# Routing logits of four token tiles: products summed on VectorE instead of transposes and products on TensorE

## The chip, the cores and the metric

One core of a Trainium2 chip runs the whole program. The metric is the device time of one execution in microseconds (us). Times inside an execution are counted from its first instruction. PE is TensorE, DVE is VectorE, ACT is ScalarE, POOL is GpSimd, and SP is the engine that issues most DMAs.

## The reference, cut to what matters

An attention with a hash mask gives x (1536 tokens of 512 numbers). A first mixture of 8 experts, weighted with Sinkhorn-normalised gates, gives a new x. The second mixture sends each token of this new x to one expert:

```python
xn = x / (np.linalg.norm(x, axis=-1, keepdims=True) + 1e-06)
en = expert_emb / (np.linalg.norm(expert_emb, axis=-1, keepdims=True) + 1e-06)
logits = xn @ en.T / tau                     # [1536, 8]
expert_idx = np.argmax(logits, axis=1)
probs = softmax(logits)
out[mask] = gate_w[mask, None] * (np.maximum(x[mask] @ w1[e], 0.0) @ w2[e])
```

The change concerns the logits of the second mixture, for tokens 0 to 511 in the kernel's tile order: 8 dot products of length 512 for each token.

## The kernel before, in words

Tokens lie in 12 tiles of 128 (TT); the first mixture works on three chunks of four tiles (CH = 3, CT = 4). The attention takes the first 250 us. Then each expert e of the first mixture does for each chunk c: the **up** product, 8 blocks f of 12 matmuls into the four PSUM banks 0 to 3 in turn; ACT takes the relu of each block (`h_hi`, L1302) and DVE the rounding rest (`h_lo`, L1737), which frees the bank. Then the **down** product, 32 pairs j of 3 matmuls into banks 4 to 7, after which DVE adds the scaled result to the four token rows (`tok`, L1800). Every fp32 product is three matmuls of rounded parts (`matmul_x3`, L476 to L480). PE holds the order of work: its instructions are written out by hand in one queue, and small products of the second mixture's routing are put between the matmuls of the last expert (e = 7).

In chunk 1 of the last expert these are the routing steps of tiles 0 to 3, whose rows are final by then. `tokens_beside` (L935) puts them before the pairs j = 7t, 7t + 3, 7t + 6 and 7t + 9 of the down product:

- `turn_token` (L909): four 128x128 transposes of the token rows into bank 0. ACT copies them to `x_t` and squares the rows for the norm (`token`, L1254).
- `token_logits` (L917): four fp32 products of `x_t` and the turned embeddings `emb_t` into bank 1.
- `token_rank` (L923): waits until DVE has chosen the expert (`s_chosen`), then two small bf16 products.
- `table_part` (L928): waits for a table cell from DVE (`s_cell`).

DVE's side is `choose` (L1646: six small instructions from the logits to the chosen expert, the running counts and a copy of the logits), then `find_cell` (L1660), then two blocks of `w2_lo` (L1723), four times (L1759 to L1767), all behind the eight `h_lo` of that chunk. On DVE, `link` (L1390) makes the engine wait for the completion of each such instruction before the next. ACT's side is, after its eight relus, `token(t, 0)` and two blocks of `w2_hi2` (L1291) for each of the four tiles (L1310 to L1313); `w2_hi2` writes the second mixture's first weights over the xt arrays.

```python
    pe.wait_ge(s_chosen, t + 1)                                  # token_rank, L924
    pe.matmul(psum[:, bank, 0:E], prior[:], chosen[:], start=True, stop=False)
```

SP loads the weights of each expert as they come free; near the end of the first mixture it issues the load of `w2_raw` (L433), and then the stores of finished token rows to `x_rows` (L435 to L453).

The last tiles (4 to 11) are routed in chunk 2 of the last expert and behind it, with the same functions. After that come the 19 or so token tiles of the second mixture (`tiles2`).

Of the kernel before, what the change touches and what calls it, by code (L numbers as in the profile page):

```python
# [13 lines left out]
P = 128  # L14
# [13 lines left out]
def program(nc, q, k, v, proj, w_gate, w1, w2, emb, tau, m2w1, m2w2, out):  # L28
# [7 lines left out]
    TT = N // P  # L36
# [36 lines left out]
    x_t = place("x_t", [P, KD, P], F32, gate_t_at)  # L73
    emb_sq = gate_t[0:E, :]
# [47 lines left out]
    assert N == 1536 and FF == 1024 and DM == 512  # L122
    left = [[dead + 4 * (kd * N + 1024)] for kd in range(4)]
# [106 lines left out]
    x_rows = nc.dram_tensor("x_rows", [N, DM], F32).ap()  # L230
    weights = nc.dram_tensor("weights", [N, 1], F32).ap()
# [3 lines left out]
    s_turned, s_copied, s_logits = sem("token_turned"), sem("token_copied"), sem("token_logits")  # L235
    s_chosen, s_rank, s_cell = sem("token_chosen"), sem("token_rank"), sem("token_cell")
# [121 lines left out]
    def _(sp):  # L358
# [65 lines left out]
        with sp.Fori(0, E - 1) as e:  # L424

            sp.wait_ge(m1.w1_lo, e + 1)
            sp.dma_start(w1_raw[:], m1.wa[e + 1]).then_inc(m1.w1_in, 16)
            sp.wait_ge(m1.w2_lo, KF * (e + 1))
            sp.dma_start(w2_raw[:], m1.wb[e + 1]).then_inc(m1.w2_in, 16)
        sp.wait_ge(m1.w1_lo, E)  # L430
        sp.dma_start(w1_raw[:], m2.wa[0]).then_inc(m2.w1_in, 16)
        sp.wait_ge(m1.w2_lo, KF * E)
        sp.dma_start(w2_raw[:], m2.wb[0]).then_inc(m2.w2_in, 16)  # L433

# [13 lines left out]
        sp.wait_ge(s_turned, 2 * CT)  # L448
# [265 lines left out]
    def _(pe):  # L714
# [194 lines left out]
        def turn_token(t, bank):  # L909
            pe.wait_ge(m1.y, (E - 1) * TT + t + 2)  # L910
            if t > 0:
                pe.wait_ge(s_squares, t)
            for kd in range(KD):
                tr = pe.transpose(psum[:, bank, kd * P:kd * P + P], tok[:, t, kd * P:kd * P + P], ident[:])
            tr.then_inc(s_turned, 1)

        def token_logits(t, bank):  # L917
            pe.wait_ge(s_copied, t + 1)
            for kd in range(KD):
                mm = pe.matmul(psum[:, bank, 0:E], x_t[:, kd, :], emb_t[:, kd, :], start=(kd == 0), stop=(kd == KD - 1))  # L920
            mm.then_inc(s_logits, 1)
# [13 lines left out]
        def tokens_beside(j, n):  # L935

            for t in range(CT):
                if j == 7 * t:
                    if t == 0:
                        pe.wait_ge(m1.h_lo, KF * n + 4 + 5)  # L940
                    turn_token(t, 0)
                if j == 7 * t + 3:
                    if t == 0:
                        pe.wait_ge(m1.h_lo, KF * n + 5 + 5)
                    token_logits(t, 1)
                if j == 7 * t + 6:
                    if t == 0:
                        pe.wait_ge(m1.h_lo, KF * n + 6 + 5)
                    token_rank(t, 2)
                if j == 7 * t + 9:  # L950
                    if t == 0:
                        pe.wait_ge(m1.h_lo, KF * n + 7 + 5)
                    table_part(t, 3)
# [122 lines left out]
        for kd in range(KD):  # L1076
            if kd % 2 == 0:
                pe.wait_ge(s_copied, TT + kd // 2)
            mm = pe.matmul(psum[:, 1, 0:E], x_t[:, kd, :], emb_t[:, kd, :], start=(kd == 0), stop=(kd == KD - 1))
# [70 lines left out]
    def _(act):  # L1150
# [103 lines left out]
        def token(t, bank):  # L1254

            if t > 0:
                act.wait_ge(s_logits, t)
            act.wait_ge(s_turned, t + 1)
            act.copy(x_t[:].rearrange("p k i -> p (k i)"), psum[:, bank, :]).then_inc(s_copied, 1)
            act.wait_ge(s_copied, t + 1)  # L1260
            act.activation(psum[:, bank, :], tok[:, t, :], ACT.Square,
                           accum_out=per_tok[:, 0, t:t + 1]).then_inc(s_squares, 1)

        def last_token():
            t = TT - 1
            act.wait_ge(s_logits, t)
            act.wait_ge(s_turn_half, 1)
            act.copy(x_t[:, 0:2, :].rearrange("p k i -> p (k i)"), psum[:, 0, 0:256]).then_inc(s_copied, 1)
            act.wait_ge(s_turned, TT)
            act.copy(x_t[:, 2:4, :].rearrange("p k i -> p (k i)"), psum[:, 7, 0:256]).then_inc(s_copied, 1)  # L1270
            act.wait_ge(s_copied, TT + 1)
            act.activation(psum[:, 0, :], tok[:, t, :], ACT.Square,
                           accum_out=per_tok[:, 0, t:t + 1]).then_inc(s_squares, 1)
# [22 lines left out]
        def expert(e, first=False, last=False):  # L1296
            for c in range(CH):
# [12 lines left out]
                if last and c == 1:  # L1310
                    for t in range(CT):
                        token(t, 0)
                        w2_hi2(0, 0, w2_raw, (2 * t, 2 * t + 1))  # L1313
# [73 lines left out]
    def _(dve):  # L1387
# [258 lines left out]
        def choose(t, bank):  # L1646

            dve.wait_ge(s_logits, t + 1)
            scores_, best = psum[:, bank, 0:E], per_tok[:, 4, t:t + 1]
# [6 lines left out]
            link(dve.tensor_copy(logit[:, t, :], scores_))  # L1656
            if t == TT - 1:
                dve.sem_inc(s_total_in, 1)

# [72 lines left out]
        def expert(e, first=False, last=False):  # L1732
            for c in range(CH):
                n = CH * e + c
                for f in range(KF):
# [5 lines left out]
                    if first and c == 1:  # L1741
# [8 lines left out]
                        if 2 <= f < 2 + CT:  # L1750
                            first_y(f - 2)
                    if last and c == 2:
# [173 lines left out]
```

## Time and profile before

| | |
|---|---|
| median of 3 runs | 1570.8 us (1570.76 to 1570.91) |
| the profiled execution's own time | 1570.5 us |
| its span, first to last instruction | 1568.6 us |
| PE busy | 1545.6 us (99%) |
| DVE busy | 686.0 us (44%) |
| ACT busy | 516.0 us (33%) |
| POOL busy | 332.3 us (21%) |
| share of the chain that ended last on PE | 96% |
| mean granted clock of PE | 0.995 |

Busy time counts an instruction from its start to its end. Neighbouring matmuls overlap in it (each lasts 0.39 us and starts 0.23 us after the last), so the distance from start to start is what a matmul costs; the same is true of two DVE instructions with no wait between them. A granted clock of 1.00 is 2.4 GHz on TensorE, 0.50 is 1.2 GHz.

### The profile page before, as it was taken

Reading aid. Unit: us, or ns where it says so; the run is one execution under the profiler, and the core shown is the slowest. Engines: PE = TensorE matmul, PEld = TensorE weight load, DVE = VectorE, ACT = ScalarE, POOL = GpSimd, SP = SyncE. Lnnn points to the kernel's source line nnn. Section 1 sums busy time; section 2 is a strip of 40 time slices with the busy share of each in tenths; the row PEclk is TensorE's granted clock in tenths of the full one; section 3 lists DMA queues with packets and bytes.
Section 4 is the critical chain, followed back from the end, with each engine's and each line's share of the span. In section 5 each row is a group of like instructions: output and inputs, shape, how many; then the busy total and the mean of one; then the engine's idle time right before and its main releaser. Section 6 shows DMA issues by size and latency. Waiting matters only on the chain.

```text
span 1568.6 us, 21673 instructions
## 1 busy us (share of the span) xinstructions
PE 1545.6 (99%) x7493; PEld 1292.6 (82%) x7494; DVE 686.0 (44%) x1242; ACT 516.0 (33%) x946; POOL 332.3 (21%) x563
## 2 busy tenths in 40 slices
PE   8999999999999999999999999999999999999997
PEld 7999997888888888888888888888888888788886
DVE  7999985423222311311322221121132255887665
ACT  6888885012111101101211111011121133676554
POOL 4565656000300300120030030012004000233222
PEclk9999999999999999999999999999999999899999
DMA  6545561101100200110110011011011122774310
GB/s 164 136 113 144 124 179 55 54 1 54 55 1 1 80 27 0 53 53 0 53 54 0 0 68 39 0 53 53 0 38 69 41 81 75 251 260 163 118 40 25
DMA packets 44775, 108.88 MB, mean 69 GB/s; under 512 B 5782, under 2 KB 7830, under 8 KB 44736
## 3 DMA queue, kind: packets, MB, share of 16 engines
q1 hardware_dynamic: 41088, 99.83, 20.4%
q0 software_dynamic: 3424, 8.14, 1.6%
q8 instruction: 24, 0.39, 0.1%
q10 hardware_dynamic: 224, 0.39, 0.1%
q14 instruction: 15, 0.12, 0.0%
HBM read 81.57 MB, written 8.13 MB: 57 GB/s over the span
## 4 chain that ended last, share of the span: by engine, by line
PE 96%; DVE 2%; ACT 1%; issue 1%; POOL 0%; DVEq 0%; POOLq 0%; ACTq 0%
PE psum L478 27%; PE psum L479 26%; PE psum L480 26%; PE psum L786 4%; PE psum L773 2%; PE psum L800 2%; PE psum L799 2%; PE psum L774 2%; PE psum L1113 1%; PE psum L754 1%; PE psum L813 1%; PE psum L920 1%; PE psum L1104 0%; ACT prob L1169 0%; DVE pt_lo L1431 0%
## 5 line engine op out<-in xcount | busy, mean ns | idle before, releaser
L1302 ACT ACTIVATE h_hi<-psum 128x512 fp32r<-128x512 f32 x192 | 114.9, 598 | 878.5 <-PE psum L480 878.5
L478 PE MATMUL psum<-w_lo,h_hi 128*128 128x512 f32 x768 | 304.4, 396 | 0.0
L479 PE MATMUL psum<-w_hi,h_hi 128*128 128x512 f32 x768 | 302.5, 394 | 0.0
L478 PE MATMUL psum<-xt_lo,w_hi 128*128 128x512 f32 x768 | 300.3, 391 | 0.0
L479 PE MATMUL psum<-xt_hi,w_hi 128*128 128x512 f32 x768 | 299.0, 389 | 0.0
L480 PE MATMUL psum<-xt_hi,w_lo 128*128 128x512 f32 x768 | 298.9, 389 | 0.0
L480 PE MATMUL psum<-w_hi,h_lo 128*128 128x512 f32 x768 | 298.5, 389 | 0.0
L1737 DVE SCALAR_TENSOR_TENSOR h_lo<-psum,h_hi 128x512 fp32r<-128x512 f32 x192 | 133.0, 693 | 351.3 <-ACT h_hi L1302 351.3
L1800 DVE SCALAR_TENSOR_TENSOR tok<-psum,route,tok 128x512 f32<-128x512 f32 x83 | 56.8, 745 | 358.6 <-PE psum L480 358.6
L509 POOL CAST w_hi<-w_raw 128x512 fp32r<-128x512 f32 x68 | 41.6, 611 | 802.0 <-PE psum L480 801.6
L480 PEld LDWEIGHTS psum<-w_hi,h_lo 128*128 128x128 f32 x768 | 144.2, 188 | 32.5
L478 PEld LDWEIGHTS psum<-w_lo,h_hi 128*128 128x128 f32 x768 | 144.2, 188 | 32.1
L480 PEld LDWEIGHTS psum<-xt_hi,w_lo 128*128 128x128 f32 x768 | 144.2, 188 | 30.1
L478 PEld LDWEIGHTS psum<-xt_lo,w_hi 128*128 128x128 f32 x768 | 144.2, 188 | 29.8
L479 PEld LDWEIGHTS psum<-xt_hi,w_hi 128*128 128x128 f32 x768 | 144.2, 188 | 29.4
L479 PEld LDWEIGHTS psum<-w_hi,h_hi 128*128 128x128 f32 x768 | 144.6, 188 | 27.4
L1431 DVE TENSOR_TENSOR pt_lo<-psum,pt_hi 128x384 fp32r<-128x384 f32 x192 | 97.5, 549 | 18.4 <-ACT pt_hi L1162 17.7
L1169 ACT ACTIVATE prob<-psum,row_bias,row_scale 128x768 f32<-128x768 f32 x96 | 95.9, 999 | 20.4 <-POOL row_bias L558 18.6
L1441 DVE TENSOR_REDUCE row_min<-psum 128x1 f32<-128x768 f32 x96 | 90.8, 947 | 1.1 <-PE psum L774 0.7
L1162 ACT CAST pt_hi<-psum 128x384 fp32r<-128x384 f32 x192 | 83.0, 486 | 14.1 <-PE psum L786 12.9
L631 POOL TENSOR_TENSOR w_lo<-w_raw,w_hi 128x512 fp32r<-128x512 f32 x64 | 82.6, 1291 | 12.5 <-issue 7.2
L786 PE MATMUL psum<-ident,prob 128*128 128x128 f32 x576 | 80.7, 275 | 2.2 <-DVE pt_lo L1431 1.7
(272 smaller groups left out, 1996.0 us busy)
## 6 DMA issues: line engine op xcount, KB each, us to landing
w_raw<-in_moe_w_dram SPq DMA_DIRECT2D x25, 2048.0 KB, 8.2
w_raw_odd<-in_moe_w_dram SPq DMA_DIRECT2D x4, 2048.0 KB, 10.3
k_hh<-k_hi SPq DMA_DIRECT2D x32, 192.0 KB, 3.0
w_raw_even<-in_moe_w_dram SPq DMA_DIRECT2D x3, 2048.0 KB, 9.2
x_rows<-tok SPq DMA_DIRECT2D x14, 256.0 KB, 2.4
k_raw<-in_k_dram SPq DMA_DIRECT2D x8, 384.0 KB, 3.1
v_raw<-in_v_dram SPq DMA_DIRECT2D x16, 192.0 KB, 3.4
q_b<-q_hi SPq DMA_DIRECT2D x16, 192.0 KB, 4.0
```

What stands on the lines that cost most here:

```text
L478: pe.matmul(acc, a[0], b[1], start=start, stop=False)
L479: pe.matmul(acc, a[0], b[0], start=False, stop=False)
L480: return pe.matmul(acc, a[1], b[0], start=False, stop=stop)
L631: pool.tensor_tensor(w2_s[1][:, f, :], w2_raw[:, f, :], w2_s[0][:, f, :].bitcast(F32), ALU.subtract).then_inc(m1.w2_lo, 1)
L786: tr = pe.transpose(psum[:, 4 + c, j * P:j * P + P], prob[par][:, 3 * c + j, :], ident[:])
L1162: act.copy(pt_hi[half][:, 3 * c:3 * c + 3, a:a + P], psum[:, 4 + c, 0:HALF].rearrange("p (j i) -> p j i", j=3)).then_inc((s_hi_a, s_hi_b)[ ...
L1169: act.activation(prob[t % 2][:].rearrange("p (c j) i -> p c (j i)", c=2), psum[:, score_bank(g, t):score_bank(g, t) + 2, 0:HALF], ACT.Exp, ...
L1302: act.activation(h_s[0][:, f, :], psum[:, f % 4, :], ACT.Relu).then_inc(m1.h_hi, 1)
L1431: dve.tensor_tensor(pt_lo[half][:, 3 * c:3 * c + 3, a:a + P], psum[:, 4 + c, 0:HALF].rearrange("p (j i) -> p j i", j=3), pt_hi[half][:, 3 ...
L1441: dve.tensor_reduce(row_min[:, c], psum[:, score_bank(g, t):score_bank(g, t) + 2, 0:HALF], AX.XY, ALU.min).then_inc(s_min, 1)
L1737: dve.scalar_tensor_tensor(h_s[1][:, f, :], psum[:, f % 4, :], 0.0, h_s[0][:, f, :].bitcast(F32), ALU.max, ALU.subtract).then_inc(m1.h_lo, 1)
L1800: dve.scalar_tensor_tensor(tok[:, tile, 0:DM], psum[:, 4 + i, :], route[:, e, tile:tile + 1], tok[:, tile, 0:DM], ALU.mult, ALU.add).then_ ...
```

## The change

The eight normalised embedding rows (16 KB, made early in the first mixture) are stored to a scratch tensor in device memory, and read back into every one of the 128 partitions (`emb_all`, 8 x 512 numbers per partition, 2 MB). `emb_all` lies over the columns of the xt arrays that chunk 0 used, so SP issues the read once the last expert's up product of chunk 0 is done. Then DVE computes, for tiles 0 to 3, each of the 8 logits with one instruction: the product of the 128 token rows with one repeated embedding row, with the sum over the 512 products put out beside it (`accum_out`). Four such linked instructions follow each `h_lo` of chunk 1 of the last expert: 32 in all. The transposes, the copies and the TensorE products of tiles 0 to 3 go; ACT's squares stay and wait for nothing of PE. ACT's `w2_hi2`, which writes over `emb_all`, waits until all four tiles' dot products are done (`s_dots`). `choose` reads the sums instead of PSUM and has no logits to copy. The counts of `s_turned`, `s_copied` and `s_logits` shift by 4.

```diff
     x_t = place("x_t", [P, KD, P], F32, gate_t_at)
+    dot_terms = x_t[:].rearrange("p k i -> p (k i)")
     emb_sq = gate_t[0:E, :]
...
     assert N == 1536 and FF == 1024 and DM == 512
+    assert 2 * KD == E
+    emb_all = place("emb_all", [P, E, N], F32, [dead])
     left = [[dead + 4 * (kd * N + 1024)] for kd in range(4)]
...
     x_rows = nc.dram_tensor("x_rows", [N, DM], F32).ap()
+    emb_rows = nc.dram_tensor("emb_rows", [E, DM], F32).ap()
     weights = nc.dram_tensor("weights", [N, 1], F32).ap()
...
     s_turned, s_copied, s_logits = sem("token_turned"), sem("token_copied"), sem("token_logits")
+    s_emb_stored, s_emb_all, s_dots = sem("emb_rows_stored"), sem("emb_broadcast_loaded"), sem("token_dots")
     s_chosen, s_rank, s_cell = sem("token_chosen"), sem("token_rank"), sem("token_cell")
...
             sp.dma_start(w2_raw[:], m1.wb[e + 1]).then_inc(m1.w2_in, 16)
+        sp.wait_ge(s_emb_ready, 1)
+        sp.dma_start(emb_rows, emb_sq).then_inc(s_emb_stored, 16)
         sp.wait_ge(m1.w1_lo, E)
...
         sp.dma_start(w2_raw[:], m2.wb[0]).then_inc(m2.w2_in, 16)
+
+        sp.wait_ge(s_emb_stored, 16)
+        sp.wait_ge(m1.up, KF * (CH * (E - 1) + 1) + 1)
+        sp.dma_start(emb_all[:, :, 0:512], emb_rows.partition_broadcast(P)).then_inc(s_emb_all, 16)
...
         sp.wait_ge(s_x_stored, 16 * 2 * CT)
-        sp.wait_ge(s_turned, 2 * CT)
+        sp.wait_ge(s_turned, CT)
         sp.wait_ge(s_squares, 2 * CT)
...
             pe.wait_ge(m1.y, (E - 1) * TT + t + 2)
-            if t > 0:
-                pe.wait_ge(s_squares, t)
+            pe.wait_ge(s_squares, t)
             for kd in range(KD):
...
         def token_logits(t, bank):
-            pe.wait_ge(s_copied, t + 1)
+            pe.wait_ge(s_copied, t - CT + 1)
             for kd in range(KD):
...
             for t in range(CT):
-                if j == 7 * t:
-                    if t == 0:
-                        pe.wait_ge(m1.h_lo, KF * n + 4 + 5)
-                    turn_token(t, 0)
-                if j == 7 * t + 3:
-                    if t == 0:
-                        pe.wait_ge(m1.h_lo, KF * n + 5 + 5)
-                    token_logits(t, 1)
                 if j == 7 * t + 6:
...
-            if t > 0:
-                act.wait_ge(s_logits, t)
-            act.wait_ge(s_turned, t + 1)
-            act.copy(x_t[:].rearrange("p k i -> p (k i)"), psum[:, bank, :]).then_inc(s_copied, 1)
-            act.wait_ge(s_copied, t + 1)
+            if t < CT:
+                act.wait_ge(m1.y, (E - 1) * TT + t + 2)
+                if t > 0:
+                    act.wait_ge(s_squares, t)
+            else:
+                if t > CT:
+                    act.wait_ge(s_logits, t - CT)
+                act.wait_ge(s_turned, t - CT + 1)
+                act.copy(x_t[:].rearrange("p k i -> p (k i)"), psum[:, bank, :]).then_inc(s_copied, 1)
+                act.wait_ge(s_copied, t - CT + 1)
             act.activation(psum[:, bank, :], tok[:, t, :], ACT.Square,
...
             t = TT - 1
-            act.wait_ge(s_logits, t)
+            act.wait_ge(s_logits, t - CT)
             act.wait_ge(s_turn_half, 1)
             act.copy(x_t[:, 0:2, :].rearrange("p k i -> p (k i)"), psum[:, 0, 0:256]).then_inc(s_copied, 1)
-            act.wait_ge(s_turned, TT)
+            act.wait_ge(s_turned, TT - CT)
             act.copy(x_t[:, 2:4, :].rearrange("p k i -> p (k i)"), psum[:, 7, 0:256]).then_inc(s_copied, 1)
-            act.wait_ge(s_copied, TT + 1)
+            act.wait_ge(s_copied, TT - CT + 1)
             act.activation(psum[:, 0, :], tok[:, t, :], ACT.Square,
...
                 if last and c == 1:
+                    act.wait_ge(m1.h_lo, KF * n + 4 + 5)
                     for t in range(CT):
                         token(t, 0)
+                        if t == 0:
+                            act.wait_ge(s_dots, CT)
                         w2_hi2(0, 0, w2_raw, (2 * t, 2 * t + 1))
...
-            dve.wait_ge(s_logits, t + 1)
-            scores_, best = psum[:, bank, 0:E], per_tok[:, 4, t:t + 1]
+            if t < CT:
+                dve.wait_ge(s_dots, t + 1)
+            else:
+                dve.wait_ge(s_logits, t - CT + 1)
+            scores_ = logit[:, t, :] if t < CT else psum[:, bank, 0:E]
+            best = per_tok[:, 4, t:t + 1]
             link(dve.tensor_reduce(best, scores_, AX.X, ALU.max))
...
             link(dve.tensor_tensor(counts[:, (t + 1) % 2, :], counts[:, t % 2, :], chosen[:], ALU.add))
-            link(dve.tensor_copy(logit[:, t, :], scores_))
+            if t >= CT:
+                link(dve.tensor_copy(logit[:, t, :], scores_))
             if t == TT - 1:
                 dve.sem_inc(s_total_in, 1)
+
+        def token_dots(t, experts):
+
+            dve.wait_ge(s_emb_all, 16)
+            dve.wait_ge(m1.y, (E - 1) * TT + t + 2)
+            for e in experts:
+                link(dve.scalar_tensor_tensor(dot_terms, tok[:, t, :], 1.0, emb_all[:, e, 0:512], ALU.mult, ALU.mult,
+                                              accum_out=logit[:, t, e:e + 1]))
+            if E - 1 in experts:
+                dve.sem_inc(s_dots, 1)
...
                             first_y(f - 2)
+                    if last and c == 1:
+                        token_dots(f // 2, range(f % 2 * E // 2, (f % 2 + 1) * E // 2))
                     if last and c == 2:
```

## Rows read from the trace of the kernel before

**Rows 1.** Busy time and clock by stretch: chunk 1 up and chunk 1 down, last expert.
```profile
core 0: us, PE busy (x) PEld busy (x) DVE busy (x) ACT busy (x) POOL busy (x), PEclk, DMA share, GB/s
1228.00:1249.80 21.80, 21.80 (x97) 17.99 (x97) 8.97 (x19) 4.19 (x7) 0.00 (x0) 1.00 0.19 72
1249.80:1278.20 28.40, 28.40 (x157) 23.25 (x155) 15.75 (x58) 9.86 (x21) 0.00 (x0) 1.00 0.01 1
```

**Rows 2.** The chain that ended last, chunk 1 down: start us, us, what.
```profile
1249.98 0.44 PE psum L914 x4
...
1252.49 0.79 PE psum L920 x8
1253.28 0.34 PE psum L478
```

**Rows 3.** PE in order of time, last expert: start us, us, engine, line.
```profile
1206.08 0.39 PE L478 MATMUL psum<-w_lo,h_hi 128*128 128x512 f32 x1
...
1228.05 0.39 PE L478 MATMUL psum<-xt_lo,w_hi 128*128 128x512 f32 x1
...
1255.06 0.40 PE L480 MATMUL psum<-w_hi,h_lo 128*128 128x512 f32 x1
1255.30 0.18 PE L925 MATMUL psum<-chosen,prior 128*128 128x8 bf16 x1
```

**Rows 4.** DVE in order of time, chunk 1 of the last expert.
```profile
1232.68 0.69 DVE L1737 SCALAR_TENSOR_TENSOR h_lo<-psum,h_hi 128x512 fp32r<-128x512 f32 x1
...
1253.31 0.17 DVE L1650 TENSOR_REDUCE per_tok<-psum 128x1 f32<-128x8 f32 x1 [1.97 <-PE psum L920]
...
1257.24 1.30 DVE L1726 TENSOR_TENSOR xt_lo<-w_raw,xt_hi 128x512 fp32r<-128x512 f32 x2
```

**Rows 5.** DVE in order of time, first expert: two unlinked instructions, then two linked ones.
```profile
320.80 0.69 DVE L1737 SCALAR_TENSOR_TENSOR h_lo<-psum,h_hi 128x512 fp32r<-128x512 f32 x1 [1.29 <-ACT h_hi L1302]
321.40 0.74 DVE L1729 TENSOR_SCALAR tok<-psum,route 128x512 f32<-128x512 f32 x1
...
332.28 0.67 DVE L1623 TENSOR_TENSOR gate_t<-emb_raw 8x512 f32<-8x512 f32 x1
332.99 0.67 DVE L1624 TENSOR_REDUCE one_col<-gate_t 8x1 f32<-8x512 f32 x1
```

**Rows 6.** DVE's groups, shapes apart: xcount, busy us, mean ns, idle before.
```profile
L1421 DVE TENSOR_TENSOR k_lo<-k_raw,k_hi 128x768 fp32r<-128x768 f32 x1 | 1.0, 957 | 0.1
L1423 DVE SCALAR_TENSOR_TENSOR q_lo<-q_raw,q_hi 128x768 fp32r<-128x768 f32 x1 | 1.0, 957 | 0.1
...
L1664 DVE TENSOR_REDUCE spot<-pick 128x1 f32<-128x8 f32 x12 | 1.9, 162 | 0.4
```

**Rows 7.** ACT in order of time: a sum's readout, two blocks of w2_hi2.
```profile
1251.67 0.19 ACT L1261 ACTIVATION_READ_ACCUMULATOR psum<-tok 128x1 f32 x1
1251.76 1.12 ACT L1294 CAST xt_hi<-w_raw 128x512 fp32r<-128x512 f32 x2
```

**Rows 8.** DVE in order of time: the last tile's choice begins.
```profile
1338.29 0.17 DVE L1650 TENSOR_REDUCE per_tok<-psum 128x1 f32<-128x8 f32 x1 [0.34 <-DVE tab L1821]
```

**Rows 9.** PE in order of time: the last tile's rank product, which waited for that choice.
```profile
1339.30 0.18 PE L925 MATMUL psum<-chosen,prior 128*128 128x8 bf16 x1 [0.92 <-DVEq L1654]
```

**Rows 10.** Busy time and clock by stretch, columns as in rows 1, after the last expert.
```profile
1338.00:1342.00 4.00, 2.46 (x18) 1.91 (x16) 2.64 (x15) 1.70 (x3) 0.84 (x4) 0.94 0.97 295
1342.00:1346.00 4.00, 2.56 (x12) 1.77 (x10) 2.59 (x11) 0.58 (x1) 0.22 (x2) 0.50 0.53 206
1346.00:1350.00 4.00, 4.00 (x10) 3.13 (x11) 2.29 (x8) 2.65 (x6) 1.44 (x3) 0.50 0.29 72
```

**Rows 11.** PE in order of time where its clock is at half and comes back.
```profile
1346.53 0.63 PE L479 MATMUL psum<-w_hi,x_hi 128*128 128x512 f32 x1
...
1351.96 0.39 PE L480 MATMUL psum<-w_hi,x_lo 128*128 128x512 f32 x1
```

**Rows 12.** DMA issues, 1195 to 1215 us: xcount, KB each, median us to landing.
```profile
w_raw<-in_moe_w_dram SPq DMA_DIRECT2D x1, 2048.0 KB, 8.4
```

More of the change, by code:

```diff
@@ L1077, in _ @@
             if kd % 2 == 0:
-                pe.wait_ge(s_copied, TT + kd // 2)
+                pe.wait_ge(s_copied, TT - CT + kd // 2)
             mm = pe.matmul(psum[:, 1, 0:E], x_t[:, kd, :], emb_t[:, kd, :], start=(kd == 0), stop=(kd == KD - 1))
```

## The prediction

> **What bounds the kernel now.** I read the page first: PE is busy for 99% of the span and the chain that ended last is 96% PE, so whatever leaves PE's queue shortens the run and whatever stops PE lengthens it. Then the busy times by stretch, for the place of the change [rows 1]: in chunk 1 of the last expert the up product takes 21.8 us and the down product 28.4 us, PE without a pause in both, clock 1.00. DVE has room there: 9.0 of 21.8 us and 15.8 of 28.4 us busy. Both products are 96 matmuls; the 6.6 us more of the second are routing work. Then the chain through the down product [rows 2], which has turns and logits on it. Then PE's and DVE's order of time [rows 3, 4], because the change moves work from one queue to the other, and the question is when each reaches the point at which PE waits for DVE: the rank product (L925) before pair 6.
>
> **Part 1, what PE loses.** For a tile, the chain has 0.44 us of turns and 0.79 us of logits, and the matmul behind the logits takes 0.34 us where one between others takes 0.23, so 0.11 more [rows 2]. That is 1.34 us; four tiles make 5.36 us, all of it on the path. Rank and table products stay.
>
> **Part 2, what DVE gets: 32 linked dot products of 512 numbers.** Neither this operation with a sum beside it nor its readout on DVE is in the trace, so I bound its distance d from start to start.
> - Below: linked instructions of 512 numbers start 0.71 us apart (332.28 to 332.99) [rows 5]. Two fp32 inputs in SBUF cost the three-operand instruction no more than a plain one: 957 ns each for 768 numbers [rows 6]. If the sum costs nothing, d is 0.71.
> - Taken: ACT shows its sum as a second instruction, the readout of 0.19 us [rows 7]. If DVE does the same, an unlinked second instruction starts 0.60 us after the first (320.80 to 321.40) [rows 5], a DVE instruction that writes one number per partition lasts 0.16 [rows 6], and the link adds the 0.04 by which 332.99 lies behind the end of 332.28 + 0.67 [rows 5]. So d is 0.60 + 0.16 + 0.04, near 0.81. I take it because a sum has to be written somewhere and the nearest engine spends an instruction on it.
> - Above: the full 0.71, plus a readout as long as ACT's 0.19, plus another 0.04: 0.94.
>
> The Trainium skill, "VectorE: DVE Perf Modes", section "Two Vector instructions with no wait between them", says that a Vector operation which also puts out its accumulator is two instructions, the operation and a read. No row here shows it on DVE; by it d would lie at 0.81 rather than at 0.71.
>
> **Part 3, when DVE is through.** Its first `h_lo` of the chunk starts at 1232.68 [rows 4], behind the sums of chunk 0 and the tables, which are unchanged. Each block f then takes 0.60 us to the first dot (not linked) and 4d: 0.60 + 3.24 = 3.84 us. A block of the up product takes PE 21.8 / 8 = 2.7 us, so from now on DVE is the slower. Eight blocks are 30.7 us, until 1263.4. From the start of a choice to PE's rank product that waited for it took 1.01 us (1338.29 to 1339.30) [rows 8, 9]. So PE can start the first rank product at 1264.4.
>
> **Part 4, where that stops PE.** Not in the up product: block f needs the bank of f - 4, freed by that block's `h_lo`. The fourth `h_lo` ends at 1232.7 + 3 x 3.84 + 0.69 = 1244.9, and PE, which began at 1228.05 [rows 3], comes to block 7 at 1228.05 + 7 x 2.7 = 1247.1. Nor do the down product's waits for `h_lo`: each block has four pairs to itself, and the last is wanted some 19 us in. But before pair 6 PE waits for the first choice, which DVE now makes only behind all 32 dots. Before, the product started at 1255.30 [rows 3]; without the first tile's turn and logits PE is there at 1255.30 - 1.34 = 1253.96. The wait is 1264.4 - 1254.0 = 10.4 us, and all of PE's queue stands behind it.
>
> **Part 5, behind the wait.** For the next tiles DVE needs, from the start of a choice to the end of its `w2_lo`, 1253.31 to 1258.54, 5.2 us with 0.9 of waiting for PE in it [rows 4]; the copy of the logits goes. PE has seven pairs between rank products, 21 matmuls of 0.23 = 4.8 us and the small products. From PE's rank product to the next choice, DVE does the cell, two `w2_lo` (1.30) and the choice, near 4.1 us, within PE's 5.1. So no second wait. ACT's `w2_hi2` waits for the dots now, but two blocks take 1.12 us [rows 7] and DVE wants them 1.8 us after the rank product; the squares need only finished rows. I cost both at nothing; if that cover went, each us would come back once per tile.
>
> **Part 6, the clock.** After the dense part ended, PE worked with gaps, and the granted clock went from 0.94 to 0.50 and stayed there into the next dense stretch [rows 10]: 1.2 instead of 2.4 GHz. There, 13 distances from start to start took 5.43 us (1346.53 to 1351.96) [rows 11] where 13 x 0.23 is 2.98: 2.5 us lost until the clock was back. A PE that does nothing for 10 us should lose it as surely. I add 2.5; the bounds are 0 (the clock stays) and 3.5 (a dense stretch of 7 us at half).
>
> **Part 7, DMAs.** SP issues two more. The 16 KB store waits for something long done. The 2 MB read of the repeated rows is issued when chunk 0's up product ends, 1206.1 [rows 3]. The load of the same size before it on that queue landed in 8.4 us [rows 12]. DVE wants the rows at 1233.3, so there are 27 us for it. Row stores behind it in SP's queue wait for rows that are final only after 1228. Nothing; without that cover each us of delay moves the first choice by one.
>
> **Sum.** -5.4 + 10.4 + 2.5 = +7.6 us on the profiled execution's 1570.5 us (1568.6 span and 1.9 around it), or 1578.1. The median of the runs shown is 0.3 above, so 1578.4. What comes after, other products and loads, starts later as a whole.
>
> By the bounds: d = 0.71 with the clock kept gives 8 x 3.44 = 27.5, rank at 1261.2, wait 7.3, so +1.9, 1572.7; with the clock lost, 1575.2. d = 0.94 gives 8 x 4.36, rank at 1268.6, wait 14.6, +9.3, and with 3.5 for the clock 1583.6.
>
> **Rivals.**
> 1. *Cheap dots.* No readout to pay, clock loss small: 1572.7 to 1574. For: [rows 5, 6]. Against: ACT's readout [rows 7] and the half clock [rows 10]. Chance 0.12.
> 2. *The dots fit: not slower.* If linked dots with a sum went at the 0.60 of unlinked instructions and the clock held, DVE would be done at 1256.7, the wait would be 3.7 us, under the 5.4 saved: 1569.1. It decides at the rank product before pair 6; below d = 0.65 the change gains, and only near 0.55 by more than 0.2%. Against: linked instructions of this width show 0.71 [rows 5]. Chance 0.05, with any error in my reading of where PE waits.
> 3. *Half rate.* The multiply with two fp32 inputs and a sum streams at half rate: 512 numbers cost what 1024 would. From 957 ns for 768 [rows 6] and 0.67 for 512 [rows 5] the slope is 0.29 us per 256, so 1.25 us, with readout and link 1.37 as d. Then a block takes 6.1 us, DVE is through at 1281.3, the rank product starts at 1282.3. PE would now stop in the up product too, but all of it ends in the same wait: 28.3 us later than 1254.0. The sum is -5.4 + 28.3 + 2.5, 1596.2. For it no row speaks; without a sum, full rate is shown. Chance 0.10. The Trainium skill, "Vector Engine (DVE) Microarchitecture Reference", section 7, says just this of such an instruction with two SBUF sources that are not bf16: it halves throughput. Rows 6 disagree where no sum is put out; with a sum nothing here shows it.
> 4. *Late rows.* The repeated read takes over 27 us, because 128 copies come from the same 16 KB. At 35 us, 8 us more: 1586. Chance 0.03.
>
> My forecast has 0.70. A measurement of this kernel can tell 0.2%, 3.1 us, from no change. Faster gets 0.04 of rival 2 (most of that is my misreading PE's wait, not its price); same gets rival 1 and the rest of rival 2, 0.13; all else is slower, 0.83. The range runs from the lowest of rival 1 to a little above my upper bound, 1572.5 to 1585, and leaves out rivals 2 and 3 and most of 4.
>
> **What would show it.** In the changed profile: PE idle some 10 us before L925 in the last expert's chunk 1, released by DVE; 32 dots at 0.81 us with short readouts behind them; `h_lo` 3.8 us apart in that up product; clock 0.50 behind the wait; no L914 or L920 in that down product; the repeated read landed before 1220. I am wrong if PE does not stop there, if the dots are under 0.65 or over 1 us apart, or if PE stops somewhere else, in the up product or at chunk 2.

## The result, and the profile after

The changed kernel takes 1576.5 us (median of 7 runs, 1575.5 to 1577.2) against 1570.9 (7 runs): ratio 1.0035, 95% interval 1.0025 to 1.0045. It is slower, by 5.5 us. Forecast were 1578.4 us, a range from 1572.5 to 1585, and slower with 0.83. One execution of one later kernel (three_overlapped) took 5339 us and is left out of its numbers.

First the waits of PE in chunk 1's down product of the last expert (line; who released it; us in total, times, longest us). Lines have moved by the edit: L935 is the rank product that was L925, L489 to L491 are the three matmuls, L1762 is `h_lo`, L1680 the dot.

```profile
PE psum L935 <- DVEq L1668: 8.4, 1, 8.4
```

Before, PE waited for nothing there. Now it stands still once, for 8.4 us, before the rank product of the first tile, and what releases it is DVE's choice. The busy times and the clock by stretch (columns as in [rows 1]):

```profile
1228.00:1249.80 21.80, 21.80 (x98) 18.06 (x97) 20.08 (x54) 4.19 (x7) 0.00 (x0) 1.00 0.19 72
1249.80:1254.00 4.20, 4.20 (x20) 3.43 (x19) 4.03 (x12) 1.21 (x3) 0.00 (x0) 1.00 0.01 2
1254.00:1258.00 4.00, 0.39 (x2) 0.00 (x0) 3.75 (x11) 0.00 (x0) 0.00 (x0) 0.82 0.00 0
1258.00:1262.00 4.00, 0.00 (x0) 0.00 (x0) 3.68 (x13) 0.31 (x1) 0.00 (x0) 0.50 0.00 0
1262.00:1266.00 4.00, 3.17 (x9) 2.54 (x10) 3.25 (x13) 4.00 (x10) 0.00 (x0) 0.50 0.01 4
1266.00:1270.00 4.00, 4.00 (x19) 3.06 (x18) 0.93 (x6) 1.79 (x5) 0.00 (x0) 0.90 0.00 0
```

In the up product DVE is busy for 20.1 of 21.8 us, where it had 9.0 [rows 1], and PE still loses nothing. Then PE is empty from 1254.4 to 1262.8, and the granted clock, 1.00 until 1254, is at 0.50 (1.2 GHz) from 1258 to beyond 1266. DVE in order of time, from the chunk's first `h_lo`, answers to [rows 4]:

```profile
1232.99 0.69 DVE L1762 SCALAR_TENSOR_TENSOR h_lo<-psum,h_hi 128x512 fp32r<-128x512 f32 x1
1233.60 0.68 DVE L1680 SCALAR_TENSOR_TENSOR x_t<-tok,emb_all 128x512 f32<-128x512 f32 x1
1234.21 0.09 DVE L1680 DVE_READ_ACCUMULATOR x_t<-tok,emb_all 128x1 f32 x1
1234.33 0.69 DVE L1680 SCALAR_TENSOR_TENSOR x_t<-tok,emb_all 128x512 f32<-128x512 f32 x1
1234.94 0.08 DVE L1680 DVE_READ_ACCUMULATOR x_t<-tok,emb_all 128x1 f32 x1
1235.06 0.69 DVE L1680 SCALAR_TENSOR_TENSOR x_t<-tok,emb_all 128x512 f32<-128x512 f32 x1
...
1236.53 0.69 DVE L1762 SCALAR_TENSOR_TENSOR h_lo<-psum,h_hi 128x512 fp32r<-128x512 f32 x1
...
1261.52 0.08 DVE L1680 DVE_READ_ACCUMULATOR x_t<-tok,emb_all 128x1 f32 x1
1261.74 0.16 DVE L1664 TENSOR_REDUCE per_tok<-logit 128x1 f32<-128x8 f32 x1
```

The sum is indeed a second instruction, 0.08 us long. A dot starts 0.73 us after the one before it (1234.33 to 1235.06), a block takes 3.54 us (1232.99 to 1236.53), and the 32 dots end at 1261.6. PE in order of time behind the wait:

```profile
1262.83 0.17 PE L935 MATMUL psum<-chosen,prior 128*128 128x8 bf16 x1 [8.44 <-DVEq L1668]
...
1266.85 0.22 PE L942 MATMUL psum<-lane_id,cell 128*96 128x128 f32 x1
...
1269.73 0.18 PE L935 MATMUL psum<-chosen,prior 128*128 128x8 bf16 x1
...
1271.95 0.22 PE L942 MATMUL psum<-lane_id,cell 128*96 128x128 f32 x1
```

Between a rank and a table product stand nine matmuls. For tile 1 that takes 2.22 us (1269.73 to 1271.95), for tile 0, at half clock, 4.02 (1262.83 to 1266.85): 1.80 us lost.

A measure serves for everything below: the **stage**, from the start of DVE's sums of chunk 0 to the start of its sums of chunk 1. It holds the up and the down product of chunk 1 and leaves out small shifts before it. It is read from one profiled execution of each kernel. Before (first line below) it is 1278.63 - 1228.25 = 50.4 us, changed (second pair) 1283.85 - 1228.55 = 55.3: 4.9 us more.

```profile
1228.25 2.73 DVE L1800 SCALAR_TENSOR_TENSOR tok<-psum,route,tok 128x512 f32<-128x512 f32 x4 [20.65 <-PE psum L480]
...
1278.63 2.73 DVE L1800 SCALAR_TENSOR_TENSOR tok<-psum,route,tok 128x512 f32<-128x512 f32 x4 [0.50 <-PE psum L480]
```
```profile
1228.55 2.73 DVE L1827 SCALAR_TENSOR_TENSOR tok<-psum,route,tok 128x512 f32<-128x512 f32 x4 [20.66 <-PE psum L491]
...
1283.85 2.73 DVE L1827 SCALAR_TENSOR_TENSOR tok<-psum,route,tok 128x512 f32<-128x512 f32 x4 [0.49 <-PE psum L491]
```

The two profiled executions differ by 4.96 us (1575.47 against 1570.51), nearly all of it in the stage (4.92). The medians differ by 0.6 us more; the profiled run is the fastest of its seven.

### The profile page after: what moved, and what is told of

Same layout as the page of the kernel before. It is cut to its first block, busy times and chain, and to the rows that moved or that the text cites. A ratio compares the mean times of both kernels' runs of the same rounds, so it can differ in the third digit from the quotient of the medians.

```text
span 1573.7 us, 21647 instructions
## 1 busy us (share of the span) xinstructions
PE 1542.4 (98%) x7445; PEld 1288.9 (82%) x7446; DVE 706.3 (45%) x1302; ACT 513.3 (33%) x942; POOL 338.5 (22%) x563
## 4 chain that ended last, share of the span: by engine, by line
PE 94%; DVE 3%; issue 1%; ACT 1%; POOL 0%; DVEq 0%; POOLq 0%; ACTq 0%
PE psum L489 26%; PE psum L490 26%; PE psum L491 26%; PE psum L797 4%; PE psum L784 2%; PE psum L811 2%; PE psum L810 2%; PE psum L785 2%; DVE x_t L1680 1%; PE psum L1115 1%; PE psum L765 1%; PE psum L824 1%; PE psum L1106 0%; PE psum L930 0%; ACT prob L1171 0%
## 5 line engine op out<-in xcount | busy, mean ns | idle before, releaser
L489 PE MATMUL psum<-w_lo,h_hi 128*128 128x512 f32 x768 | 304.4, 396 | 0.0
L489 PE MATMUL psum<-xt_lo,w_hi 128*128 128x512 f32 x768 | 300.2, 391 | 0.0
L491 PE MATMUL psum<-w_hi,h_lo 128*128 128x512 f32 x768 | 299.0, 389 | 0.0
L491 PE MATMUL psum<-xt_hi,w_lo 128*128 128x512 f32 x768 | 298.9, 389 | 0.0
L1762 DVE SCALAR_TENSOR_TENSOR h_lo<-psum,h_hi 128x512 fp32r<-128x512 f32 x192 | 132.8, 692 | 339.1 <-ACT h_hi L1309 338.5
L489 PEld LDWEIGHTS psum<-w_lo,h_hi 128*128 128x128 f32 x768 | 144.6, 188 | 32.6
L491 PEld LDWEIGHTS psum<-w_hi,h_lo 128*128 128x128 f32 x768 | 144.6, 188 | 32.6
L491 PEld LDWEIGHTS psum<-xt_hi,w_lo 128*128 128x128 f32 x768 | 144.2, 188 | 30.0
L489 PEld LDWEIGHTS psum<-xt_lo,w_hi 128*128 128x128 f32 x768 | 144.2, 188 | 29.9
```

Source lines behind the costliest of these rows:

```text
L489: pe.matmul(acc, a[0], b[1], start=start, stop=False)
L491: return pe.matmul(acc, a[1], b[0], start=False, stop=stop)
L1762: dve.scalar_tensor_tensor(h_s[1][:, f, :], psum[:, f % 4, :], 0.0, h_s[0][:, f, :].bitcast(F32), ALU.max, ALU.subtract).then_inc(m1.h_lo, 1)
```

## Experiments

Stage and total in one table; the theory is that each tile taken off PE saves 1.34 us, that DVE's dots are paid only as a wait in front of the first product that needs DVE, and that the clock adds to a long wait. The rival to all of it is that dots, reads or bookkeeping cost something of their own. In `nodots` DVE computes no dots; the kernels named after two or three tiles compute dots on DVE for so many of the four, and route the others on PE as before.

| kernel | stage us | PE's wait us | median us | ratio to before (95%) |
|---|---|---|---|---|
| before | 50.4 | none | 1570.9 | |
| changed | 55.3 | 8.4 | 1576.5 | 1.0035 (1.0025 to 1.0045) |
| nodots | 44.9 | none | 1540.8 (other work) | |
| two_tiles | 47.9 | none | 1568.3 | 0.9988 (0.9979 to 0.9997) |
| three_tiles | 49.0 | 2.6 | 1569.7 | 0.9999 (0.9990 to 1.0008) |
| filled_wait | 53.5 | 0.9 | 1574.1 | 1.0024 (1.0014 to 1.0033) |
| early_choice_three | 50.6 | 2.6 | 1570.5 | 0.9999 (0.9990 to 1.0008) |
| overlapped_dots | 52.4 | 5.5 | 1572.9 | 1.0012 (1.0003 to 1.0021) |
| three_tiles_filled | 49.0 | 0.5 | 1568.9 | 0.9990 (0.9981 to 0.9999) |
| three_overlapped | 46.8 | 0.4 | 1567.5 | 0.9979 (0.9970 to 0.9988) |
| three_overlapped_late | 46.6 | none | 1566.7 | 0.9971 (0.9959 to 0.9983) |

The chips' own kernels before lay at 1570.6 to 1571.1, so a few tenths between medians of different rows mean nothing; the ratios are against runs on the same chip. What a kernel's median gains or loses against before on its own chip follows its stage within 0.9 us in every row but `nodots`.

Two places outside the stage differ from profile to profile. In the first 50 us the mean granted clock is 1.00 in seven kernels and 0.97 in four (two_tiles, overlapped_dots and the last two), and in these four the stage starts at 1229.7 to 1230.2 instead of 1228.3 to 1228.8. The edits do not touch the code that runs there. From 1340 to 1360, around [rows 10], it is 0.74 in before, changed and overlapped_dots, where 289.9 to 290.1 us follow the stage, and 0.83 in the others but `nodots`, where 288.4 to 289.4 us follow. So a total moves by 0.5 to 2 us from clock losses that have nothing to do with PE's wait in the stage.

### The dots left out

```diff
         def token_dots(t, experts):
             dve.wait_ge(s_emb_all, 16)
             dve.wait_ge(m1.y, (E - 1) * TT + t + 2)
-            for e in experts:
-                link(dve.scalar_tensor_tensor(dot_terms, tok[:, t, :], 1.0, emb_all[:, e, 0:512], ALU.mult, ALU.mult,
-                                              accum_out=logit[:, t, e:e + 1]))
```

> The 32 dot products are left out; everything else of the change stays, and the first four tiles are routed by what lies in their logits (those of the first mixture's gate), so the number of tiles of the second mixture can differ by one or so: the stage is read, not only the total. Theory (TensorE's saving is whole, DVE's dots alone give it back): PE never stops in chunk 1 of the last expert, its down product falls from 28.4 to 23.0 us (4 x 1.34 less), clock 1.00 throughout, total near 1565.5 us. Rival (a part of the turns and logits was hidden, or the new DMAs and waits cost something of their own): the down product takes over 24 us, or PE stops somewhere.

Measured: no wait of PE in the stage, and DVE's sums of chunk 1 start at 1273.69, those of chunk 0 at 1228.79.

```profile
1228.79 2.73 DVE L1824 SCALAR_TENSOR_TENSOR tok<-psum,route,tok 128x512 f32<-128x512 f32 x4 [20.65 <-PE psum L491]
...
1273.69 2.73 DVE L1824 SCALAR_TENSOR_TENSOR tok<-psum,route,tok 128x512 f32<-128x512 f32 x4 [0.49 <-PE psum L491]
```

The stage is 44.9 us, 5.5 under before; 5.4 were predicted. So PE's saving is whole, and the changed waits cost nothing. The read of 2 MB (1206.6 to 1214.1 in the changed kernel) lies ahead of the stage; PE takes 22.17 us from the start of chunk 0's down product to DVE's sums of chunk 0 both before (1206.08 to 1228.25) and changed (1206.38 to 1228.55), so it costs nothing either. The total, 1540.8, was expected near 1565.5 and is no measure here: other routing makes the second mixture's work another. I had written that this might differ by a tile or so. The traces show two: 15 issues of `out_dram` rows instead of 17, and 120 up-product matmuls of each kind behind 1340 us instead of 136, 8 to a tile. The 25 us are then 12 us a tile.

### Dots for two tiles, for three tiles

```diff
+    ND = 2
...
             for t in range(CT):
+                if t >= ND and j == 7 * t:
+                    turn_token(t, 0)
+                if t >= ND and j == 7 * t + 3:
+                    token_logits(t, 1)
...
-                        token_dots(f // 2, range(f % 2 * E // 2, (f % 2 + 1) * E // 2))
+                        todo = range(ND * f, ND * f + ND)
+                        for t in sorted({i // E for i in todo}):
+                            token_dots(t, [i % E for i in todo if i // E == t])
```

(and ND in the place of CT in the counts of the semaphores; ND = 3 for the other.)

> Dots on DVE for tiles 0 and 1 alone, two behind each h_lo; tiles 2 and 3 are turned and multiplied on PE as before. Theory: a block on DVE takes 0.61 + 2 x 0.735 = 2.1 us, under PE's 2.7, so DVE is done before the rank product; no wait, no loss of clock; 2 x 1.34 = 2.7 us less than before: 1568.2 us, ratio 0.9983. Rival (dots beside h_lo cost PE something whatever their number, or the read of the repeated rows does): 1571 us or more.

> Dots on DVE for tiles 0 to 2, three behind each h_lo; tile 3 on PE as before. Theory: 0.61 + 3 x 0.735 = 2.8 us a block, dots done at 1255.6, rank product possible at 1256.8, PE there at 1254.2: 2.6 us of wait against 4.0 saved: 1569.4 us if the clock stays through so short a stop, 1571.2 if it falls as it did behind the 8.4 us stop. Rival (the wait is a matter of 4 tiles' bookkeeping, not of the number of dots): a wait of 8 us still.

With two tiles PE waits for nothing, and the stage is 2.5 us under before (2.7 expected); the total gains 0.12%, a little less than the 0.17% expected, whose value lies inside the interval. With three, the wait is as computed:

```profile
PE psum L936 <- DVEq L1673: 2.6, 1, 2.6
```

The stage loses 1.4 us against before, which is -4.0 + 2.6 (expected -1.4). In this profile the clock stayed at 1.00. Over its 11 runs the kernel lies between 1567.8 and 1571.8 us, and the runs above 1570.5 have a mean clock of 0.993 or 0.994 where those below have 0.995 to 0.997. The kernel before spreads nearly as much on the same chip, 1569.1 to 1571.8 us at clocks from 0.994 to 0.997, so this grouping does not say where the clock was lost. That the wait goes from 8.4 to 2.6 to none with the number of tiles shows that it is a matter of how many dots DVE has, not of the change's bookkeeping; the rivals fall.

### Matmuls where PE would wait

```diff
                     if t == 0:
+                        pe.wait_ge(m1.h_lo, KF * n + 5 + 5)
+                        for i in range(11):
+                            matmul_x3(pe, psum[:, 1, :], [h[:, 0, 0:P] for h in h_s], [w[:, 0, :] for w in w2_s], True, True)
                         pe.wait_ge(m1.h_lo, KF * n + 6 + 5)
                     token_rank(t, 2)
```

> The change, with 33 matmuls of 512 columns (7.6 us of dense work whose result nobody reads) put on PE ahead of the first rank product, in bank 1, where PE would stand still. Theory (the half clock behind the stop costs 1.8 us of the 5.5): the granted clock stays at 1.00, the rank product starts at the same time, 1262.8, and the total is 1.8 us under the changed kernel's: 1574.7 us, with less spread from run to run. Rival (the clock costs nothing that PE did not have to wait for anyway): 1576.5 us as before the filling.

```profile
1254.00:1258.00 4.00, 4.00 (x19) 3.31 (x18) 3.75 (x11) 0.00 (x0) 0.00 (x0) 1.00 0.00 0
1258.00:1262.00 4.00, 3.91 (x18) 2.87 (x16) 3.68 (x13) 0.36 (x1) 0.00 (x0) 1.00 0.00 0
1262.00:1266.00 4.00, 3.22 (x16) 2.70 (x17) 3.25 (x13) 4.00 (x11) 0.00 (x0) 1.00 0.00 0
```
```profile
1262.78 0.17 PE L935 MATMUL psum<-chosen,prior 128*128 128x8 bf16 x1 [0.87 <-DVEq L1671]
...
1264.98 0.22 PE L942 MATMUL psum<-lane_id,cell 128*96 128x128 f32 x1
```

The rank product starts where it did, 1262.8; the clock stays at 1.00; rank to table takes 2.20 us instead of 4.02. The stage is 1.8 us shorter than the changed kernel's, as the theory has it: PE does 33 more matmuls and is sooner through. The intervals of the two ratios overlap (1.0014 to 1.0033 and 1.0025 to 1.0045), so the total alone would not show it; the stage and the clock do. The spread did not narrow as I expected: 1572.9 to 1575.7, where the changed kernel had 1575.5 to 1577.2.

The same was tried where the stop is short (three tiles, nine matmuls in the same place):

> Three tiles on DVE with late choices, and 9 unread matmuls (2.1 us) where PE would stand still for 2.6. Theory (the clock falls in some executions behind the 2.6 us stop, which spreads the three-tile kernel over 1567.8 to 1571.8): the same stage length as without them where the clock held, 49.0 us, all runs in the lower group, median near 1568.3, clock 0.996 in every run. Rival (the spread has another cause): the same spread and median as without them.

Stage 49.0 us as expected, median 1568.9 (near 1568.3 expected) instead of 1569.7, no run above 1570.3 where there had been five. But the two sets ran on different chips, the intervals of their ratios overlap, and the runs' clocks still go from 0.994 to 0.997, as those of the kernel before do. The expected clock of 0.996 in every run did not come. So it is not shown that this stop makes any part of the spread. The two places outside the stage, the first 50 us and 1340 to 1360, differ by 0.5 to 2 us between profiles and are the likelier source.

### Choices ahead of time

```diff
                             token_dots(t, [i % E for i in todo if i // E == t])
+                        if f == 5:
+                            choose(0, 1)
...
-                        choose(t, 1)
+                        if t >= ND:
+                            choose(t, 1)
                         find_cell(t, 2)
+                        if t + 1 < ND:
+                            choose(t + 1, 1)
```

> Three tiles on DVE; tile 0's choice goes ahead, behind the dots of block 5, and the choices of tiles 1 and 2 ahead of the w2_lo of the tile before. Theory (PE waits only for the first choice being last in DVE's row): no wait over 0.3 us in chunk 1's down product, 3 x 1.34 = 4.0 us less than before, 47.9 - 1.3 = 46.5 us from chunk 0's sums to chunk 1's (50.4 before, 49.0 with three tiles and late choices), total 1566.7 against 1570.7, ratio 0.9975, and no spread from the clock. Rival (DVE is simply full: the wait moves to the second tile's rank product): 49.0 us again, ratio 0.9990.

```profile
PE psum L943 <- DVEq L1718: 2.6, 1, 2.6
```
```profile
1258.00:1262.00 4.00, 2.67 (x10) 2.18 (x11) 3.23 (x12) 4.00 (x10) 0.00 (x0) 0.85 0.00 0
1262.00:1266.00 4.00, 4.00 (x16) 2.90 (x15) 1.77 (x9) 0.04 (x1) 0.00 (x0) 0.73 0.00 0
```

A miss, for both theories as I had put them. The rank product no longer waits, but the table product three pairs on (L943) does, for 2.6 us: it wants the first tile's cell, and `find_cell` stands behind all dots as before. The wait was not bound to the choice; it belongs to whichever product first needs anything that DVE does behind the dots. And in this execution the clock did fall at a stop of 2.6 us, which makes the stage 50.6 instead of 49.0. The twelve matmuls from the first table product to the second rank product take 4.20 us where three_tiles has 2.88, and the nine behind them 2.51 instead of 2.22: together the 1.6 us.

### Dots that overlap

```diff
-                link(dve.scalar_tensor_tensor(dot_terms, tok[:, t, :], 1.0, emb_all[:, e, 0:512], ALU.mult, ALU.mult,
-                                              accum_out=logit[:, t, e:e + 1]))
+                chain[0] += 1
+                dve.scalar_tensor_tensor(dot_half[e % 2], tok[:, t, :], 1.0, emb_all[:, e, 0:512], ALU.mult, ALU.mult,
+                                         accum_out=logit[:, t, e:e + 1]).then_inc(s_chain, 1)
+                dve.wait_ge(s_chain, chain[0] if e == experts[-1] else chain[0] - 1)
```

(`dot_half` are the two halves of `x_t`, which take the products in bf16 in turn; the sums stay fp32. The last dot of each block is still linked.)

> The change, with each dot linked to the one before the last and not to the last (two halves of x_t take the products in bf16 in turn; the sums stay fp32). Theory (d = 0.735 is 0.61 of the pitch that unlinked instructions show, 0.08 readout and 0.04 link): d falls to 0.69 or 0.70, the 32 dots end 1.0 to 1.4 us sooner, the wait is 7.2 us, total 1575.2. Rival (the readout drains the engine, and the link was hidden behind it): d stays at 0.73, total 1576.5.

```profile
1235.23 0.68 DVE L1682 SCALAR_TENSOR_TENSOR x_t<-tok,emb_all 128x512 bf16<-128x512 f32 x1
1235.83 0.08 DVE L1682 DVE_READ_ACCUMULATOR x_t<-tok,emb_all 128x1 f32 x1
1235.83 0.69 DVE L1682 SCALAR_TENSOR_TENSOR x_t<-tok,emb_all 128x512 bf16<-128x512 f32 x1
...
1237.06 0.69 DVE L1682 SCALAR_TENSOR_TENSOR x_t<-tok,emb_all 128x512 bf16<-128x512 f32 x1
1237.67 0.08 DVE L1682 DVE_READ_ACCUMULATOR x_t<-tok,emb_all 128x1 f32 x1
1237.79 0.69 DVE L1765 SCALAR_TENSOR_TENSOR h_lo<-psum,h_hi 128x512 fp32r<-128x512 f32 x1
```

Better than both theories: a dot now takes 0.61 us from start to start (1235.23 to 1237.06 for three). The readout begins with the next dot and costs nothing. So the 0.12 us above 0.61 is what the link costs, by making the next dot wait for the end of the readout. The bf16 products are not the reason: the fourth dot, which writes bf16 too but is linked, still takes 0.73 us to the next instruction (1237.06 to 1237.79). The stage falls by 2.9 us against the changed kernel, with the wait 8.4 to 5.5; 24 dots that are 0.12 shorter make the same 2.9. I had expected 1.0 to 1.4 us, because I still counted the readout as work.

### A version that beats both

Faster than the kernel before and than the changed one should be the two findings together: three tiles, three dots a block with a wait only for the dot before the last, across tiles too. A block then takes 0.61 + 3 x 0.61 = 2.44 us, under PE's 2.7.

```diff
+            for i in dots:
+                t, e = divmod(i, E)
...
+                dve.scalar_tensor_tensor(dot_half[i % 2], tok[:, t, :], 1.0, emb_all[:, e, 0:512], ALU.mult, ALU.mult,
+                                         accum_out=logit[:, t, e:e + 1]).then_inc(s_chain, 1)
+                dve.wait_ge(s_chain, chain[0] if done and i == dots[-1] else chain[0] - 1)
...
-                        token_dots(f // 2, range(f % 2 * E // 2, (f % 2 + 1) * E // 2))
+                        token_dots(range(ND * f, ND * f + ND))
```

> Three tiles on DVE, three dots a block, each dot linked only to the one before the last. Theory (a dot costs DVE 0.61 so, and three of them with an h_lo take 0.61 + 3 x 0.61 = 2.45 to 2.6 us a block, under PE's 2.7): DVE, which starts the chunk behind, is done at about 1254 us of the changed kernel's clock, the first rank product waits 0.5 to 1 us, the stage from chunk 0's sums to chunk 1's takes 46.9 to 47.4 us (50.4 before, 55.3 changed), the clock holds in every run, and the total is 3.0 to 3.5 us under before: ratio 0.9978 to 0.9981. Rival (the dots' traffic or DVE's bunching costs PE a wait elsewhere, as the early choices did at the table product): stage of 48.5 us or more.

```profile
1234.47 0.69 DVE L1773 SCALAR_TENSOR_TENSOR h_lo<-psum,h_hi 128x512 fp32r<-128x512 f32 x1
...
1236.91 0.69 DVE L1773 SCALAR_TENSOR_TENSOR h_lo<-psum,h_hi 128x512 fp32r<-128x512 f32 x1
...
1252.49 0.69 DVE L1773 SCALAR_TENSOR_TENSOR h_lo<-psum,h_hi 128x512 fp32r<-128x512 f32 x1 [0.25 <-ACT h_hi L1315]
```
```profile
1256.25 0.17 PE L937 MATMUL psum<-chosen,prior 128*128 128x8 bf16 x1 [0.38 <-DVEq L1674]
```

Blocks of 2.44 us; the last `h_lo` waits for ACT again, so DVE has caught up with PE by then. PE waits 0.4 us. Ratio 0.9979 (0.9970 to 0.9988), as expected. The stage, 46.8 us, is 0.1 under the range expected. The clock does not hold in every run as expected: the mean clocks go from 0.994 to 0.996, as before. With rank and table products one pair later (7t + 7 and 7t + 10):

> The same, with the rank and table products one pair later (7t + 7 and 7t + 10). Theory: the rest of the wait, 0.5 to 1 us, goes, the stage takes 46.4 us, all four savings of the three tiles (4.0 us) arrive: ratio 0.9974. Rival (what PE gains, DVE loses at the end of the stage, where its last w2_lo now lie later and the sums of chunk 1 behind them): no faster than the kernel without the shift.

No wait of PE, stage 46.6 us (46.4 expected), ratio 0.9971 (0.9959 to 0.9983): the fastest kernel of the study. The two intervals overlap, so that the later place is better than the earlier is shown by the profiles alone.

```profile
1276.45 2.73 DVE L1838 SCALAR_TENSOR_TENSOR tok<-psum,route,tok 128x512 f32<-128x512 f32 x4 [0.22 <-DVE table L1733]
```

The rival was right in part: the sums now wait for DVE's own copy of the table and start 0.85 us behind the start of PE's last matmul of the down product (1275.60), where they started 0.43 behind it. So of the 0.6 us that PE gained in this product, the stage shows 0.2.

## Why the prediction was right, point by point

- **Part 1, PE's saving.** Predicted 5.36 us, measured 5.5 (the stage without dots). Right.
- **Part 2, the price of a dot.** Predicted 0.81, measured 0.73, inside the bounds of 0.71 and 0.94. The form of the sum was right and one term of it mis-sized: the readout lasts 0.08 and not the 0.16 that I took from DVE's small instructions, and 0.61 + 0.08 + 0.04 is 0.73. What the part did not see is that the readout is no work of DVE's for as long as nobody waits for its end. It is the link behind it that costs, 0.12 us, and without the link a dot is at the 0.61 of the unlinked instructions in [rows 5]. Part 2 quoted the Trainium skill ("VectorE: DVE Perf Modes", "Two Vector instructions with no wait between them") for two instructions where a sum is put out; the 32 readouts in the changed profile agree.
- **Part 3, when DVE is through.** Blocks of 3.84 us predicted, 3.57 measured on average ((1261.6 - 1233.0) / 8): 2.1 us less over eight. The block's start was 0.3 late (1232.99 for 1232.68), and from the dots' end to the rank product it took 1.2 instead of 1.0. The first rank product was possible at 1262.8 instead of 1264.4.
- **Part 4, where it stops PE.** Right in place (the first rank product, and nowhere in the up product) and in number, one stop. Its length, 10.4 predicted and 8.6 measured (from 0.23 us behind the start of the last matmul at 1254.01 to 1262.83), follows from part 2. What this part missed does not show in this kernel: the table product behind the rank product is bound to the dots just as much, as the early choices showed.
- **Part 5, behind the wait.** Right: no second wait. ACT's late `w2_hi2` held nobody up: its first two blocks ended at 1262.83, and DVE came to them at 1264.78.
- **Part 6, the clock.** It fell, as predicted. It cost 1.8 us and not 2.5; the half clock lasted until about 1266.8 (mean 0.59 from 1266 to 1267, 1.00 behind it), 4.0 us into the dense stretch, where [rows 10, 11] had shown more than five. The price came from one place of the kernel and was carried over to another; that it would be within 0.7 us was not given by the argument. Of the 5.5 us, the fill shows 1.8 to be the clock's. The stop itself would have made -5.4 + 8.6 = +3.2.
- **Part 7, the DMAs.** The read landed in 7.5 us, at 1214.1, 19 us before it was wanted. Rival 4 falls.
- **Sum.** Predicted +7.6; measured -5.4 + 8.6 + 1.8 = +5.0 in the profiles and 5.5 in the medians. The terms that were too high are the wait, through the dot (by 1.8 us), and the clock (by 0.7).
- **The rivals.** Rival 1 was nearly right in its price for the dot (0.73 for 0.71) and wrong on the clock. Rival 2 falls as it stood: linked dots do not go at 0.60. Its question is only in part answered. With three of four dots in a block unlinked, four tiles still do not gain (1.0012), because DVE is 5.5 us late and the clock falls: rank to table takes 4.02 us there too (1261.54 to 1265.56), 1.8 lost. Without that loss the stage would be 50.6 against 50.4 before, an estimate; no run has four tiles with overlapped dots and the wait filled, or with all dots unlinked. Rival 3, half rate, falls: a dot of 512 fp32 numbers lasts 0.69 us, as long as an `h_lo`, one source of which lies in PSUM. Here the Trainium skill ("Vector Engine (DVE) Microarchitecture Reference", section 7), which has such an instruction with two SBUF sources that are not bf16 at half throughput, and this trace differ: half rate would have made it about 1.25 us. The trace decides.

## What to carry to other kernels

Work moved off the bounding engine is worth its price only up to the point at which the receiving engine is late for the next thing the bounding engine waits for; count the receiver's time to that wait, not its idle share, and move as many pieces as fit (here three tiles of four: -0.29% instead of +0.35%). Where a chain of instructions is linked only for safety, give it two buffers and wait for the instruction before the last; here that took a dot from 0.73 to 0.61 us. And when a wait is moved away, look at once at the next product behind it, which may hang on the same row of work.

## What the runs showed of the hardware that I had not expected

- DVE's readout of a sum, 0.08 us, starts together with the next instruction where nothing is linked (both at 1235.83), so an unlinked sum is free: 0.61 us a dot, as without a sum.
- A stop of TensorE of 2.6 us left the granted clock at 1.00 in one execution (three_tiles) and dropped it in another (early_choice_three, down to 0.73 in a stretch of 4 us, 1.6 us of time). The stop lay 2.3 us later there, behind other work, and which of these decides is not shown. Work of no use in the gap kept the clock up and made the stage 1.8 us shorter where the stop was 8.4 us.
- With the same code, the mean clock of the first 50 us is 1.00 in some executions and 0.97 in others, and the rest of the kernel then starts 1 to 2 us later.
